# The fold's first product: its first 128 columns loaded and rounded apart, the other factor's first block loaded in halves on two queues

## The reference

```python
a = softmax(scale * q @ k.T + bias, masked)      # per head
x = (a @ v), heads side by side                  # 1536 x 512
for e in range(4):
    h = maximum(x @ w1[e], 0)
    out += p[:, e:e+1] * (h @ w2[e])
a = out @ moe2_w1
b = out @ moe2_w2
h = a * b @ w3                                   # w3: 1024 x 1024
y = h @ w_out                                    # w_out: 1024 x 512
```

## Time and profile before

| | |
|---|---|
| median of 3 runs | 800.34 us (798.87 to 801.72) |
| the profiled execution | 803.45 us, span 801.4 us |
| PE busy | 785.4 us of the span, 98% |
| granted TensorE clock, mean over the span | 0.999 |
| POOL, DVE, ACT busy | 69%, 61%, 43% |
| PE idle before its first instruction | 1.07 us |
| PE idle between the warm-up and the first product | 0.54 us |

### The profile page before, as it was taken

The page is one execution under the profiler, slowest core; times in us unless marked ns, Lnnn a source line. Parts: engine busy times, 40 slices in busy tenths (PEclk is TensorE's granted clock), DMA queues, the critical chain, the costliest instruction groups (busy, mean ns, idle before and its releaser), DMA issues.

```text
span 801.4 us, 14261 instructions
## 1 busy us (share of the span) xinstructions
PE 785.4 (98%) x4726; PEld 747.5 (93%) x4726; DVE 491.1 (61%) x1061; ACT 341.0 (43%) x733; POOL 550.8 (69%) x515
## 2 busy tenths in 40 slices
PE   9999999999999999999999999999999999999997
PEld 7677779999999999999988899899999999999997
DVE  6896687513624533634878548448568568777741
ACT  5476785424522531533443317317317327333320
POOL 3489898698893894797797618947947938943330
PEclk9999999999999999999999999999999999999999
DMA  7943565867684585575367993383482482448773
GB/s 242 405 159 114 192 228 209 343 263 282 225 327 165 197 317 199 200 267 206 131 267 254 375 349 129 119 259 116 121 279 94 131 280 83 132 171 298 254 244 116
DMA packets 61406, 175.13 MB, mean 219 GB/s; under 512 B 7040, under 2 KB 14224, under 8 KB 61328
## 3 DMA queue, kind: packets, MB, share of 16 engines
q1 hardware_dynamic: 58816, 168.74, 58.9%
q10 hardware_dynamic: 2448, 5.38, 2.0%
q0 software_dynamic: 64, 0.03, 0.1%
HBM read 115.89 MB, written 58.22 MB: 217 GB/s over the span
## 4 chain that ended last, share of the span: by engine, by line
PE 74%; POOL 12%; DMA 6%; DVE 2%; SPq 2%; issue 2%; ACT 1%; DVEq 0%; POOLq 0%; ACTq 0%
PE bank L50 23%; PE bank L52 22%; PE bank L51 22%; POOL al L1380 3%; PE bank L627 3%; DMA al<-splits 3%; PE bank L637 3%; PE bank L656 3%; POOL sl L2177 2%; POOL bl L1466 1%; DMA x<-x_second 1%; POOL al L1302 1%; POOL al L1292 1%; DMA fold_wo_raw<-m_out 1%; DMA fold_mt_raw<-m3t 1%
## 5 line engine op out<-in xcount | busy, mean ns | idle before, releaser
L50 PE MATMUL bank<-bh,ah 128*128 128x384 f32 x672 | 226.2, 337 | 3.2 <-DVE parts L2279 1.4
L52 PE MATMUL bank<-bh,al 128*128 128x384 f32 x672 | 224.7, 334 | 0.0
L51 PE MATMUL bank<-bl,ah 128*128 128x384 f32 x672 | 224.6, 334 | 0.0
L50 PEld LDWEIGHTS bank<-bh,ah 128*128 128x128 f32 x672 | 126.1, 188 | 7.2 <-issue 3.9
L51 PEld LDWEIGHTS bank<-bl,ah 128*128 128x128 f32 x672 | 126.2, 188 | 0.0
L52 PEld LDWEIGHTS bank<-bh,al 128*128 128x128 f32 x672 | 126.2, 188 | 0.0
L50 PE MATMUL bank<-sh,ah 128*128 128x384 f32 x336 | 113.1, 337 | 5.6 <-DMA al<-splits 1.7
L52 PE MATMUL bank<-sh,al 128*128 128x384 f32 x336 | 112.4, 334 | 0.0
L51 PE MATMUL bank<-sl,ah 128*128 128x384 f32 x336 | 112.3, 334 | 0.0
L50 PE MATMUL bank<-hh,w2h 128*128 128x384 f32 x256 | 85.5, 334 | 0.0
L51 PE MATMUL bank<-hl,w2h 128*128 128x384 f32 x256 | 85.5, 334 | 0.0
(11 more groups left out here) (192 smaller groups left out, 1573.9 us busy)
## 6 DMA issues: line engine op xcount, KB each, us to landing
raw<-weights SPq DMA_DIRECT2D x56, 512.0 KB, 3.6
splits<-ah SPq DMA_DIRECT2D x28, 896.0 KB, 4.1
splits<-al SPq DMA_DIRECT2D x28, 896.0 KB, 6.4
ah<-splits SPq DMA_DIRECT2D x64, 256.0 KB, 3.4
al<-splits SPq DMA_DIRECT2D x64, 256.0 KB, 4.2
ah<-splits SPq DMA_DIRECT2D x32, 384.0 KB, 4.9
al<-splits SPq DMA_DIRECT2D x32, 384.0 KB, 6.1
k<-k SPq DMA_DIRECT2D x8, 704.0 KB, 6.9
```

The costliest lines, as they stand in the source:

```text
L50: nc.tensor.matmul(out, wh, xh, start=start, stop=False, skip_group_check=adds_on)
L51: nc.tensor.matmul(out, wh, xl, start=False, stop=False, skip_group_check=adds_on)
L52: return nc.tensor.matmul(out, wl, xh, start=False, stop=stop, skip_group_check=adds_on)
```

## The change

The first tile's first 128 columns, all that the first matmul (f = 0) takes from it, become a transfer of their own (64 KB), first on SP's queue, and a rounding of their own on ACT. The other 384 columns of that half (192 KB) go on ACT's queue. Block 0 of w_out (256 KB) goes in halves of 128 KB: columns 0 to 255 first on ACT's queue, columns 256 to 511 second on SP's. The first matmul waits for the 128 rounded columns; the second waits for the rest. Both halves of block 0 count on one semaphore.

```diff
@@ first_loads (SP)
+        sp.dma_start(self.mt_raw[0][:, 0:P], self.m3t[0][:, 0:P]).then_inc(self.column_loaded, 16)
+        c = slice(PIECE // 2, PIECE)
+        sp.dma_start(self.wo_raw[:, c], self.m_out[:, c]).then_inc(self.wo_loaded[0], 16)
         for j in range(2):
             for s in range(2):
+                if j == s == 0:
+                    continue
                 c = self.half(s)
                 sp.dma_start(self.mt_raw[j][:, c], self.m3t[j][:, c]).then_inc(
                     (self.mt_loaded if j else self.first_loaded)[s], 16)
@@ scalar (ACT)
-        for s in range(2):
-            c = self.half(s)
-            act.dma_start(self.wo_raw[:, c], self.m_out[:, c]).then_inc(self.wo_loaded[s], 16)
+        c = slice(0, PIECE // 2)
+        act.dma_start(self.wo_raw[:, c], self.m_out[:, c]).then_inc(self.wo_loaded[0], 16)
+        rest = slice(P, PIECE)
+        act.dma_start(self.mt_raw[0][:, rest], self.m3t[0][:, rest]).then_inc(self.first_loaded[0], 16)
+        c = self.half(1)
+        act.dma_start(self.wo_raw[:, c], self.m_out[:, c]).then_inc(self.wo_loaded[1], 16)
+        act.wait_ge(self.column_loaded, 16)
+        self.nc.scalar.activation(self.mt_h[0][:, 0:P], self.mt_raw[0][:, 0:P], ACT.Copy).then_inc(self.column_hi, 1)
         for g in range(4):
-            j, c = g // 2, self.half(g % 2)
+            j, c = g // 2, self.half(g % 2) if g else rest
             act.wait_ge((self.mt_loaded if j else self.first_loaded)[g % 2], 16)
             self.nc.scalar.activation(self.mt_h[j][:, c], self.mt_raw[j][:, c], ACT.Copy).then_inc(self.first_hi, 1)
@@ first_wo, first_low (DVE)
-        dve.wait_ge(self.wo_loaded[0], 16)
+        dve.wait_ge(self.wo_loaded[0], 32)
...
+        if g == 0:
+            dve.wait_ge(self.column_hi, 1)
         dve.wait_ge(self.first_hi, g + 1)
@@ first_step (PE)
             if n == 0:
-                pe.wait_ge(self.first_hi, 1)
+                pe.wait_ge(self.column_hi, 1)
                 pe.wait_ge(self.wo_first, 1)
...
             for f in range(self.WIDE):
+                if n == 0 and f == 1:
+                    pe.wait_ge(self.first_hi, 1)
```

More of the change, by code:

```diff
@@ L109, in __init__ @@
         self.first_loaded = [sem(f"fold_first_loaded{s}") for s in range(2)]
+        self.column_loaded = sem("fold_column_loaded")
+        self.column_hi = sem("fold_column_hi")
         self.mt_loaded = [sem(f"fold_mt_loaded{s}") for s in range(4)]
```

## The result

| | before | changed |
|---|---|---|
| median of 17 runs each | 800.31 us (798.21 to 804.99) | 803.96 us (800.16 to 808.38) |
| the profiled execution, its span | 803.45, 801.4 | 804.83, 802.8 |
| ratio, 95% interval | | 1.0040 [1.0022, 1.0059] |

The account below looks back on a forecast made before the run. PE bounds the kernel, busy 785.4 of 801.4 us. First product 0.48 us earlier, 0.3 kept to g = 1, 0.1 to g = 2, 0 from g = 4, plus d = 0.1: 800.4 us, range 798.3 to 802.1.

Parts of the forecast that it names:

- The first product: PE's first matmul at the start: inputs land sooner, so it starts at about 5.2 us, 0.48 us earlier, at most 0.54.
- PE is in its warm-up until 5.14: Start of PE: the warm-up ends at 5.14 us, so the first matmul cannot start sooner, though inputs are ready.
- head start: PE from the second matmul on: 0.3 us ahead, that matmul at about 5.6 instead of 5.91.
- before anything lands: free: ACT's start: a third issue costs 0.45 us and pushes the table load's end to 3.41, before any landing, so no cost.
- ACT's durations: Column rounding on ACT at the start: 0.31 us for 128 columns and 0.52 for 384.
- g = 1: PE's entry to inner block 1: 0.42 us of cover keeps the 0.3 us gain, if block 1 lands as before.
- tile 0's second half is held back: Rival, chance 0.18: SP's third transfer lands at 6.9 instead of 6.0, PE enters g = 1 at 8.9; 801.0 to 801.6.
- From 9.59 us on this is a chain of landings, DVE and POOL: From block 2 of w_out on: later waits hang on landings, DVE and POOL; PE's start is not in it.
- g = 2: PE's entry to inner block 2: ready at 10.95, entered at 11.20; only about 0.1 of the 0.3 us is left.
- g = 4: PE's entry to inner block 4: it already waited 0.27 us, so an earlier PE only waits longer; gain becomes 0.
- d = +0.1: Shift of the landings from block 2 of w_out on: 0.1 us later, for 256 more, shorter rows.
- The gap filled: Rival, chance 0.12: landings up to 0.9 us earlier (799.4), or DVE escapes POOL, 1.5 us in all (798.8).

Follow-up runs that it names:

- e14: The kernel before, unchanged, run once more for another profiled execution: 798.58 us, with 800.86 for before beside it.
- e13: The kernel before, unchanged, run once for another profiled execution: 804.21 us, with 800.86 for before beside it.
- e1: Kernel before with only the column split: tile 0's first 128 columns first, other 384 second on SP, block 0 whole on ACT; 801.0 us, ratio 1.0008.
- e9: Kernel before with the gates' 24 KB transfer moved from POOL to second on SP's queue; 801.67 us, ratio 1.0016 [1.0005, 1.0028].
- e15: The kernel of e9 again (gates' 24 KB second on SP's queue), one execution: 802.12 us, with 800.86 for before beside it.
- e8: Changed kernel with POOL's two small transfers issued by SP instead, behind block 3 of w_out; 801.45 us, ratio 1.0012.
- e2: Kernel before with only block 0 of w_out in two halves (ACT, SP), tile 0's first half whole; 801.12 us, ratio 1.0009.
- e16: The changed kernel, unaltered, for a third profiled execution, one execution: 802.77 us, with 800.86 for before beside it.
- e10: The changed kernel, unaltered, run again for a second profiled execution; 803.03 us, ratio 1.0034 [1.0017, 1.0051].
- e5: Kernel before, with PE made to wait ahead of g = 1 until block 4 of w_out has landed; 805.19 us, ratio 1.0050.
- e7: Kernel before with POOL's two small transfers issued by SP instead, behind block 3 of w_out; 800.27 us, ratio 0.9989 [0.9975, 1.0003].
- e11: Kernel before, with PE made to wait ahead of g = 1 until block 3 of w_out has landed; 801.99 us, ratio 1.0019.
- e6: Changed kernel with six blank 128-column PE matmuls between the first block's passes and g = 1; 803.65 us, ratio 1.0029.
- e3: Changed kernel with POOL's two small transfers issued later, behind POOL's tables (2.87 and 3.57 us); 801.99 us, ratio 1.0012.

## Why the prediction was wrong

**The first product, "5.2 (0.48 us earlier)": wrong, and it cost little.** The inputs came sooner than I worked out, above all the column: it was rounded by 3.77, where I had 4.78; block 0 by 4.70, where I had 4.87. What failed is the bound "PE is in its warm-up until 5.14". The end of the warm-up is no fixed time. Its matmuls start 0.21 us apart at first and 0.11 apart later, and the change of pace comes at another time in each execution: at 3.92 us in before's first trace, and only among the first products, at 6.49 and 7.29, in e14 and e13. The granted clock column reads 1.00 all the while; that this is the clock is read from the pace, which is the 0.43 us of the stretches with 0.50 for matmuls of 512 columns. The traces' records of the granted clock begin at those same times. In all traces, whatever was loaded, the first product started between 5.44 and 5.80. The 0.3 us of head start that the rest of the sum passed on was never there. And the table load, over "before anything lands: free", was in the way: the column had landed at 3.16 and ACT began at 3.46. The warm-up hid that.

**ACT's durations: right.** 0.31 for 128 columns and 0.52 for 384, as worked out.

**The step that failed is g = 1:** "The cover of 0.42 us holds a PE that is 0.3 ahead, if block 1 lands as before. It is third on ACT's queue now, yet the bytes for tile 0 and blocks 0 and 1 are the same 1024 KB, all of them at the head of two queues." Equal bytes did not mean equal landings. As third on SP's queue instead of second the half came 1.6 to 2.0 us later with the bytes unchanged (e1) or 24 KB more (e9, e15), behind packets of POOL's that held the DMA engines. Both third transfers of the changed kernel, SP's half tile and ACT's block 1, landed late together (9.99 and 10.18 in its first trace, 6.04 and 6.36 before). In place of a cover of 0.42 us there was a wait of 3.52.

**The rival "tile 0's second half is held back": right in mechanism, and mis-sized twice.** It had a landing at 6.9, g = 1 at 8.9 and 801.0 to 801.6. Measured were 8.4 to 10.0, 10.5 to 12.1 and 803.96. Its mechanism, that the hole falls just ahead of SP's third transfer, is what e9's packets show. The first reason for the size is that I took the 0.9 us of missing bytes for the delay. A transfer waits for the last of its sixteen parts, and single parts came much later than the rest (below), 1.6 us behind the middle one even where POOL had nothing in the stream (e8). The second is that it priced a wait as its length less the waits behind it. That is right for e1, e2, e9 and e16, where 1.5 to 2.3 us later landings left -0.39 to +0.43 at 344 us. It is wrong beyond: with 2.8 to 4.3 us idle the clock falls, and 3.1 to 4.4 us stay (e10, the changed kernel, e5). I gave this rival 0.18 and said that to be slower by 0.3% "it would need more than twice its upper end". That ratio was mis-worked too, since 2.4 is 1.8 times its 1.3. The 3.65 us came from landings later than it had and from the half clock, a term that the sum did not have.

**"From 9.59 us on this is a chain of landings, DVE and POOL. PE's start is not in it": right only while PE is not late.** After, ACT's rounding of tile 2 waited 3.46 us for PE (the row at 16.80). PE then had no waits left at g = 4, g = 6 and tile 4.

**g = 2, g = 4 and d = +0.1** can't be judged as such, since g = 1 moved everything. In e1 and e2, where g = 1 was 1.2 to 1.7 us late, the shift later was +0.08 and -0.39: that the waits behind absorb a short lateness was right. That they would absorb a head start can't be said, since no execution had one.

**The gap filled: not by this change, but shown possible.** By e7 the rival's mechanism and its 1.5 us are real at 344 us, and not measurable at the end.

**Two slips that change nothing.** The prediction calls the 4.1 us of the first landing twice what the Trainium skill's formula gives (DMA: Bandwidth & Descriptors, section "Anatomy of one DMA"). By that formula, 2.0 us plus bytes over 436 GB/s, the estimate for 256 KB is 2.6 us, so they are 1.6 times as much. The 1536 KB and the six and eight transfers "ahead of block 2" count block 2 itself; the differences that d was worked out from stay.

**What stays open.** Why the last parts of a third transfer straggle, and what the third place costs where no packet of POOL's stands in the stream at all: the transfers of e9 with both of POOL's taken off it were not run. How much of the whole is the start's is open too: e9, e11, e1, e2 and e8 are about where before's first trace is at 344 us (-0.39 to +0.14), and yet their medians lie 0.1 to 1.5 us above before, in e9 and e11 with an interval above 1. Single traces can't settle it: between 435 us and the end they change by -2.8 (e8) to +1.7 us (e6) against the first trace of before.

## What to carry to other kernels

Splitting a transfer to have its first part sooner moves everything behind it one place down its queue. At the start of this program what became third landed 1.5 to 2 us later with at most 128 KB more ahead, where it stood behind a small transfer of GpSimd's: count places, look up who needs the transfer that becomes third, and look at the busy share of each DMA queue in the stretch, not only at GB/s. Before making PE's inputs earlier, see whether PE can take them, in more than one execution: here the wait that was to be shortened stood in 3 of 18 traces. And price a wait of PE twice, once as time that later waits absorb and once with the granted clock: at g = 1 a wait of 1.8 us cost next to nothing and one of 2.8 us cost all of itself, while a wait of 1.76 us elsewhere did bring the clock down (e13).

## What the runs showed of the hardware

**One transfer, sixteen landings.** The landing events of tile 0's second half, counted in the traces, in us:

| | first | 8th | 15th | 16th |
|---|---|---|---|---|
| before | 5.32 | 5.59 | 5.97 | 6.04 |
| e9 | 6.97 | 7.20 | 7.57 | 7.64 |
| changed | 5.33 | 6.82 | 9.52 | 9.99 |
| e10 | 5.35 | 6.93 | 7.58 | 9.38 |
| e16 | 5.41 | 6.70 | 7.59 | 8.39 |
| e3 | 4.91 | 5.73 | 7.68 | 7.83 |
| e8 | 5.50 | 6.07 | 7.60 | 7.66 |

In e9 all are late alike, behind POOL's packets. In the changed kernel with POOL's transfers in place the first comes as early as before and the middle one 1.1 to 1.3 us later; then one to three parts straggle by another 0.8 to 2.5 us, and the semaphore's wait is for the last of them. These traces also have as many packets of about a microsecond or more on POOL's queue as stragglers (three of 0.96 to 1.07 us, one of 1.76, one of 0.99). That the ones make the others is likely and not shown. In e3 and e8 the middle one is 0.1 and 0.5 us late, and only the last three to five straggle.

**A hole from small packets.** POOL's two small transfers (2 and 24 KB) make a hole in the other queues' stream some 3 to 4 us after their issue. The sixteen 128-byte packets of the 2 KB one took 0.35 to 1.56 us each in before, 0.95 to 1.59 in e9; taking both off POOL fills the hole (e7), and the medians show no gain from that.

**The clock.** At g = 1 the granted clock fell to 0.50, the lower level of 1.2 GHz, at 12.20 in the changed kernel (3.52 us idle until 12.12), at 12.51 in e10 (2.77 idle until 11.50) and at 12.61 in e5 (4.31 idle until 13.11), each time for 3.4 us. It stayed at 1.00 behind 1.83 us in e16, but fell behind waits of 1.75 and 1.76 us that ended at 455.0 and 460.9 us in e6 and e13. The length of the wait alone doesn't decide. The rise at the start came at 3.9 us in before's first trace and at 7.3 in e13's. The Trainium skill (TensorE: Matmul & The Clock Gate, section "What's actually happening") tells of both, the fall after idleness and a rise at the start whose moment varies from run to run; the traces agree. It puts that variation at half a microsecond either way, and the traces, with 3.9 to 7.3 us, show more.
